# One move for both first units' x, tables and weight splits at other places, three runs of unread matmuls, and the last output groups two and two

## The chip, the cores and the metric

The kernel runs on one core of a Trainium2 chip. The metric is the device time of one execution in microseconds (us); less is better. Engines are TensorE (PE in the profile; PEld is its weight load), VectorE (DVE), ScalarE (ACT), GpSimd (POOL) and SyncE (SP), which only issues DMAs here.

## The reference

A gated linear attention over 4 batches, 8 heads, 768 tokens and head size 48; then a mixture of 4 experts over its 3072 x 384 output; then a gated feed-forward layer.

```python
for t in range(S):
    state = alpha[:, :, t, :, None] * state + np.einsum('bhd,bhe->bhde', k[:, :, t], v[:, :, t])
    y[:, :, t] = np.einsum('bhd,bhde->bhe', q[:, :, t], state)
...
p = domain_probs / (domain_probs.sum(-1, keepdims=True) + 1e-09)
for e in range(E):                       # E = 4, w1[e] 384 x 1024, w2[e] 1024 x 384
    h = np.maximum(x @ w1[e], 0.0)
    out += p[:, e:e + 1] * (h @ w2[e])
...
h = x @ w_in                             # 384 x 2048
g = h - np.tanh(h)
return (g @ w_out).astype(np.float32)    # 2048 x 384
```

## The kernel before

**Attention.** Tokens are cut into 12 units u of 256 tokens; each is worked through in 17 steps (`attention(u, step)`). Products of decays at three levels (`tabulate`, nine tables on the way) scale queries (`spread_queries`, `spread_distant`, `rotate`) and keys (`raise_keys`), so that TensorE can form the scores of a chunk (`diagonal`, `scores(u, level, half)`). DVE picks the valid ones with copy_predicated (`pick`). `turn` transposes keys, `deltas` forms each chunk's part of the state, `states` on DVE adds them up in time, `carry_own` copies the states beside the values, and `attend` gives the outputs, which are x for the next stage. Scores and tables lie in two sets of buffers: set 1 (names ending in b) is for unit 1 alone, set 0 for all others. Units 0 and 1 (`AHEAD = 2`) run ahead of everything; the rest are interleaved with the feed-forward part, unit 2m+2 from slot 0 of block m and unit 2m+3 from slot 16. Steps are one to a slot.

**x.** An fp32 product is made from three fp32r products of high and low parts, so each operand is split: the high part is a copy (ScalarE: `high_x`, `split_high`, `hidden_high`), the low one a subtraction (DVE: `low_x`, `split_low`, `hidden_low`; GpSimd makes some of the weights'). `attend` leaves 128 of 384 features of x in 16-row pieces at the wrong place; they go through the buffer XS and are moved by DMAs (`move`, `move_half`), three pieces kt with two halves of the rows each.

**Feed-forward.** Tokens go in 6 blocks m of 512; each has 32 slots s of the experts and 16 slots f of the last layer. A slot is `first` (x times a 384 x 128 weight block, nine products of 512 columns) and, four slots later, `second` (the hidden block times the next weights). DVE scales the hidden block (`scale`). In the last layer `cube` and ScalarE's `functions` form g, and `second2` adds into four output tiles t. Weights come from DRAM by SP (`stage(g)`, four staging buffers WS), are split into the ring RG, and saved for the later blocks (`save`).

**Order.** Each engine's program is written out by hand; engines meet by semaphores. `w_low` counts the weight splits' low parts in order, whoever makes them: splits 0 and 1 are GpSimd's, 2 to 5 DVE's, then 6 and on GpSimd's. GpSimd waits with split 6 until `w_low` is 6:

```python
def split_low(g):                         # on GpSimd
    if g == LEAD + 2:                     # LEAD = 4
        pool.wait_ge(w_low, g)
    pool.wait_ge(w_high, g + 1)
...
def attention(u, step):                   # on GpSimd
    if step in (3, 6, 9):
        raise_keys(u, step // 3 - 1)
```

TensorE's `scores(u, level, half)` with level 1 wait for `keys_up`, which `raise_keys` counts; `first(m, s)` waits for `scaled` of slot s - 2; `scores(2, 0, 1)` waits for the picks of `scores(2, 0, 0)`.

Of the kernel before, what the change touches and what calls it, by code (L numbers as in the profile page):

```python
# [7 lines left out]
fp32 = mybir.dt.float32  # L8
f32r = mybir.dt.float32r
# [8 lines left out]
P = 128  # L18
CH = 64
# [66 lines left out]
def own(u):  # L86

    return int(u == 1)
# [6 lines left out]
def turn_of(u):  # L95

    return len(same_set(u))
# [21 lines left out]


def carried_at(u):
    return 4 * (turn_of(u) + 1)
# [18 lines left out]
def program(nc, qka_d, v_d, dp_d, w1_d, w2_d, win_d, wout_d, mask_d, ones_d, ident_d, out_d):  # L141
    ctx = ExitStack()
    with ctx:
# [45 lines left out]
        T64 = [place(f"T64_{n}", CHUNKS) for n in range(2)]  # L189
        XS = [place("XS", 2 * UT, f32r), place("XSb", 2 * UT, f32r)]  # L190

# [13 lines left out]
        def sems(name):  # L205
            return sem(name), sem(name + "_b")
# [17 lines left out]
        x_low = sems("x_low")  # L224
        moved = [sems(f"moved{j}") for j in range(KT)]

# [82 lines left out]
        def to_move(u, j, hh):  # L309

            src = XS[own(u)][CH * hh + SPARE * j:CH * hh + SPARE * (j + 1), :].rearrange("p (h t) -> p h t", h=2)
            dst = x_tile(u)[CH * hh + D:CH * hh + CH, :, j, x_tokens(u)]
            return dst.bitcast(fp32), src.bitcast(fp32)

        def state_slot(u, c):
# [26 lines left out]
        def _(sp):  # L342
# [12 lines left out]
            def move(u):  # L355
                for j in (2, 0, 1):
                    sp.wait_ge(x_low[own(u)], 3 * turn_of(u) + (2 if j == 2 else 3))
                    for hh in range(1 if u == 1 else 2):
                        dst, src = to_move(u, j, hh)
                        sp.dma_start(dst, src).then_inc(moved[j][own(u)], 16)  # L360

# [90 lines left out]
            for g in range(2):  # L452
                stage(g + STAGES)
            move(0)
            move(1)
            for g in range(2, LEAD):
# [24 lines left out]
        def _(pe):  # L481
# [89 lines left out]
            def attend(u, n):  # L571
# [10 lines left out]
                last.then_inc(filled[own(u)], 1)  # L582

            def attention(u, step):
                if step == 0:
                    diagonal(u)
                if step in (1, 2):
                    scores(u, 0, step - 1)
                if step in (4, 5):
                    scores(u, 1, step - 4)  # L590
                if step in (7, 8):
                    scores(u, 2, step - 7)
                if step == 10:
# [25 lines left out]
            def first_product(m, g, out, x_moved=False, x_mixed=False):  # L619
                order = (2, 0, 1) if x_moved else (0, 1, 2)  # L620
                for kt in order:
                    if x_moved:
                        for u in (2 * m, 2 * m + 1):
                            pe.wait_ge(moved[kt][own(u)], 32 * turn_of(u) + 32)
                    if x_mixed:
                        pe.wait_ge(x2_low, KT * m + kt + 1)
                    nc.tensor.matmul(out, w1(g, 0, kt), x_part(m, 0, kt), start=(kt == order[0]), stop=False)  # L627
                    nc.tensor.matmul(out, w1(g, 0, kt), x_part(m, 1, kt), start=False, stop=False)  # L628
                    last = nc.tensor.matmul(out, w1(g, 1, kt), x_part(m, 0, kt), start=False, stop=(kt == order[-1]))  # L629
                last.then_inc(hid, 1)  # L630
# [73 lines left out]
            pe.wait_ge(prob_step, E + 2)  # L704
            nc.tensor.transpose(bank[3][0:E * NTB * TT, 0:P], prob[:, :], ident[:, :]).then_inc(prob_turned, 1)
            deltas(1, 0)
            deltas(1, 1)
            attend(0, 0)
            pe.wait_ge(prob_laid, 1)
            attend(0, 1)  # L710
            attend(1, 0)
            attend(1, 1)
            diagonal(AHEAD)
            for m in range(NTB):
                for s in range(SLOTS1):
# [15 lines left out]
                for f in range(SLOTS2):  # L731
                    first2(m, f)
                    if f >= LEAD:
                        second2(m, f - LEAD)
            for t in range(TT):
                for f in range(SLOTS2 - LEAD, SLOTS2):
                    second2(NTB - 1, f, [t])
# [3 lines left out]
        def _(act):  # L741
# [52 lines left out]
            def high_x(u):  # L794
                x, t = x_tile(u), x_tokens(u)
                if u // 2 >= 2:
                    act.wait_ge(hid, SLOTS * (u // 2 - 1))
                act.wait_ge(filled[own(u)], filled_at(u, 18))
                if turn_of(u):
                    for j in range(KT):  # L800
                        act.wait_ge(moved[j][own(u)], 32 * turn_of(u))
                nc.scalar.activation(XS[own(u)][:, 0:UT], fill_bank(u, 18)[:, UT:2 * UT], ACT.Copy).then_inc(x_high[own(u)], 1)
                nc.scalar.activation(x[:, 0, 2, t], fill_bank(u, 18)[:, 0:UT], ACT.Copy).then_inc(x_high[own(u)], 1)
                act.wait_ge(filled[own(u)], filled_at(u, 19))
                nc.scalar.activation(x[:, 0, 0:2, t], fill_bank(u, 19)[:, :].rearrange("p (a t) -> p a t", a=2),
                                     ACT.Copy).then_inc(x_high[own(u)], 1)

            def move_half(u):
                for j in (2, 0, 1):
                    act.wait_ge(x_low[own(u)], 3 * turn_of(u) + (2 if j == 2 else 3))  # L810
                    dst, src = to_move(u, j, 1)
                    act.dma_start(dst, src).then_inc(moved[j][own(u)], 16)

# [75 lines left out]
            high_x(1)  # L889
            move_half(1)  # L890
            split_high(LEAD)
# [24 lines left out]
        def _(dve):  # L916
# [95 lines left out]
            def low_x(u):  # L1012
                x, t = x_tile(u), x_tokens(u)
                dve.wait_ge(x_high[own(u)], 3 * turn_of(u) + 2)
                nc.vector.tensor_tensor(XS[own(u)][:, UT:2 * UT], fill_bank(u, 18)[:, UT:2 * UT], XS[own(u)][:, 0:UT].bitcast(fp32),
                                        ALU.subtract).then_inc(x_low[own(u)], 1)
# [180 lines left out]
            rotate(AHEAD, 0)  # L1197
            split_low(LEAD)
            split_low(LEAD + 1)
            for m in range(NTB):  # L1200
                for s in range(SLOTS1):
# [5 lines left out]
                    for u, step in units_at(m, s):  # L1207
                        attention(u, step)
                low_x2(m)
                for f in range(SLOTS2):  # L1210
# [9 lines left out]
        def _(pool):  # L1220
# [24 lines left out]

            def prepare(u):
                n = turn_of(u)
# [4 lines left out]
                tabulate(u, 0, 1)  # L1252
                spread_queries(u)
                spread_distant(u)
                tabulate(u, 1, 9)
# [34 lines left out]
            split_low(1)  # L1290
            pool.wait_ge(carried[1], carried_at(1))
            prepare(2)
            split_low(LEAD + 2)
# [45 lines left out]
```

## Time and profile before

| | us |
|---|---|
| median of 3 runs | 1391.01 |
| lowest and highest | 1390.82, 1391.07 |
| the profiled execution | 1391.59 |
| its span in the trace | 1389.8 |
| PE busy | 1346.7 (97%) |
| DVE busy | 873.0 (63%) |
| ACT busy | 559.8 (40%) |
| POOL busy | 274.0 (20%) |

All times of the trace count from the start of the span. A row of a timeline has the start, the time from the first start to the last end of the instructions merged in it, engine, line, operation and tile, their number, and in brackets how long the engine was idle before it and what released it. Records of fp32 products come in pairs, so x64 are 32 products.

### The profile page before, as it was taken

What the parts mean: (1) busy time and instruction counts of PE and PEld (TensorE: products, weight loads), DVE (VectorE), ACT (ScalarE), POOL (GpSimd) and SP (SyncE); (2) the same over time, 40 slices, a digit from 0 to 9 for tenths busy, and PEclk for the clock granted to TensorE, in tenths of its full rate; (3) what the DMA queues carried; (4) which work ended last, traced back from release to release, by engine and by line L of the source; (5) the groups of instructions that cost most, each with busy time, mean ns of one, the idle gap of its engine ahead of it and who ended that gap; (6) DMA issues with size and microseconds to landing.
All of it is one profiled execution on the core that took longest, in us unless ns stands there. A gap on an engine that the chain in (4) does not pass through costs nothing.

```text
span 1389.8 us, 25813 instructions
## 1 busy us (share of the span) xinstructions
PE 1346.7 (97%) x10177; PEld 1130.4 (81%) x10177; DVE 873.0 (63%) x1763; ACT 559.8 (40%) x1002; POOL 274.0 (20%) x272
## 2 busy tenths in 40 slices
PE   3599999999999999999999999999999999999998
PEld 3578788988878888878898887898887889888887
DVE  8884855994654875465687565497556378333385
ACT  1525346843213751313662323374231376111185
POOL 4566655004022001313001403000221000000000
PEclk8799999999999999999999999999999999999999
DMA  7389696966655656565755655665664465655552
GB/s 214 90 307 319 235 327 232 325 211 220 205 197 190 233 181 219 177 211 193 241 183 180 219 195 194 206 229 169 221 204 166 159 221 189 217 191 195 193 192 70
DMA packets 104968, 289.08 MB, mean 208 GB/s; under 512 B 10032, under 2 KB 64912, under 8 KB 104848
## 3 DMA queue, kind: packets, MB, share of 16 engines
q1 hardware_dynamic: 104704, 287.33, 61.6%
q8 instruction: 81, 1.33, 0.4%
q14 instruction: 39, 0.32, 0.1%
q10 hardware_dynamic: 144, 0.10, 0.0%
HBM read 242.52 MB, written 42.52 MB: 205 GB/s over the span
## 4 chain that ended last, share of the span: by engine, by line
PE 88%; DVE 6%; issue 3%; POOL 2%; ACT 1%; DMA 0%; DVEq 0%; POOLq 0%; ACTq 0%
PE bank L627 14%; PE bank L628 13%; PE bank L629 13%; PE bank L652 9%; PE bank L653 9%; PE bank L654 9%; PE bank L676 4%; PE bank L678 4%; PE bank L677 4%; PE bank L542 3%; PE bank L579 1%; PE bank L566 1%; DVE RG L1110 1%; DVE GG L1080 1%; PE bank L520 1%
## 5 line engine op out<-in xcount | busy, mean ns | idle before, releaser
L839 ACT ACTIVATE HH<-GG 128x512 fp32r<-128x512 f32 x192 | 121.2, 631 | 654.5 <-PE bank L654 529.1
L627 PE MATMUL bank<-XB,RG 128*128 128x512 f32 x864 | 349.8, 405 | 3.8 <-DMA XB<-XSb 3.5
L628 PE MATMUL bank<-XB,RG 128*128 128x512 f32 x864 | 340.7, 394 | 0.0
L629 PE MATMUL bank<-XB,RG 128*128 128x512 f32 x864 | 339.7, 393 | 0.0
L1053 DVE SCALAR_TENSOR_TENSOR GG<-bank,PB 128x512 f32<-128x512 f32 x192 | 133.3, 695 | 318.1 <-PE bank L629 317.9
L652 PE MATMUL bank<-HH,RG 128*128 128x512 f32 x576 | 224.6, 390 | 0.0
L653 PE MATMUL bank<-HH,RG 128*128 128x512 f32 x576 | 224.5, 390 | 0.0
L654 PE MATMUL bank<-HL,RG 128*128 128x512 f32 x576 | 224.3, 389 | 0.0
L1264 POOL TENSOR_TENSOR KU<-KU,TOT 128x256 f32<-128x256 f32 x88 | 68.5, 805 | 704.2 <-PE bank L542 704.2
L627 PEld LDWEIGHTS bank<-XB,RG 128*128 128x128 f32 x864 | 162.9, 189 | 44.6 <-issue 3.6
L629 PEld LDWEIGHTS bank<-XB,RG 128*128 128x128 f32 x864 | 162.9, 189 | 35.4
L628 PEld LDWEIGHTS bank<-XB,RG 128*128 128x128 f32 x864 | 163.1, 189 | 28.7
L1059 DVE TENSOR_TENSOR HL<-GG,HH 128x512 fp32r<-128x512 f32 x192 | 159.1, 828 | 8.9 <-ACT HH L839 8.8
L949 DVE COPY_PREDICATED SC<-masks,bank 128x192 f32<-128x192 int32 (+2 forms) x396 | 98.8, 357 | 67.5 <-PE bank L542 67.2
L676 PE MATMUL bank<-RG,HH 128*128 128x384 f32 x384 | 129.7, 338 | 1.5 <-DVE HL L1089 1.4
L678 PE MATMUL bank<-RG,HL 128*128 128x384 f32 x384 | 129.7, 338 | 0.0
L677 PE MATMUL bank<-RG,HH 128*128 128x384 f32 x384 | 129.1, 336 | 0.0
L652 PEld LDWEIGHTS bank<-HH,RG 128*128 128x128 f32 x576 | 108.2, 188 | 23.0
L654 PEld LDWEIGHTS bank<-HL,RG 128*128 128x128 f32 x576 | 108.2, 188 | 22.5
L653 PEld LDWEIGHTS bank<-HH,RG 128*128 128x128 f32 x576 | 108.2, 188 | 22.5
L1076 DVE TENSOR_TENSOR GG<-SQ,bank 128x512 f32<-128x512 f32 x96 | 65.7, 684 | 39.7 <-ACT TH L849 39.7
L848 ACT ACTIVATE SQ<-bank 128x512 f32<-128x512 f32 x96 | 57.1, 595 | 67.4 <-PE bank L629 66.3
(129 smaller groups left out, 1654.4 us busy)
## 6 DMA issues: line engine op xcount, KB each, us to landing
RG<-scratch SPq DMA_DIRECT2D x240, 768.0 KB, 4.3
scratch<-RG SPq DMA_DIRECT2D x48, 768.0 KB, 5.2
VS<-vp SPq DMA_DIRECT2D x11, 768.0 KB, 6.0
WS<-w SPq DMA_DIRECT2D x32, 192.0 KB, 3.1
PB<-probs SPq DMA_DIRECT2D x6, 1024.0 KB, 6.8
AU<-qka SPq DMA_DIRECT2D x11, 512.0 KB, 5.4
R<-qka SPq DMA_DIRECT2D x11, 512.0 KB, 5.2
KU<-qka SPq DMA_DIRECT2D x11, 512.0 KB, 6.2
```

Of the source, the lines that this page charges most:

```text
L627: nc.tensor.matmul(out, w1(g, 0, kt), x_part(m, 0, kt), start=(kt == order[0]), stop=False)
L628: nc.tensor.matmul(out, w1(g, 0, kt), x_part(m, 1, kt), start=False, stop=False)
L629: last = nc.tensor.matmul(out, w1(g, 1, kt), x_part(m, 0, kt), start=False, stop=(kt == order[-1]))
L652: nc.tensor.matmul(out, w2(g, 0)[:, c], HH[:, h_slot(g)], start=(s == 0), stop=False)
L653: nc.tensor.matmul(out, w2(g, 1)[:, c], HH[:, h_slot(g)], start=False, stop=False)
L654: return nc.tensor.matmul(out, w2(g, 0)[:, c], HL[:, h_slot(g)], start=False, stop=(s == SLOTS1 - 1))
L676: nc.tensor.matmul(out, HH[:, h], w2(g, 0), start=(f == 0), stop=False)
L677: nc.tensor.matmul(out, HH[:, h], w2(g, 1), start=False, stop=False)
L678: last = nc.tensor.matmul(out, HL[:, h], w2(g, 0), start=False, stop=(f == SLOTS2 - 1))
L839: nc.scalar.activation(HH[:, h_slot(g)], GG[:, h_slot(g)], ACT.Copy).then_inc(high, 1)
L1053: nc.vector.scalar_tensor_tensor(GG[:, h_slot(g)], h_bank[s % 2][:, :], 0.0, PB[:, e * TB:e * TB + TB], op0=ALU.max, op1=ALU.mult).then_in ...
L1059: nc.vector.tensor_tensor(HL[:, h_slot(g)], GG[:, h_slot(g)], HH[:, h_slot(g)].bitcast(fp32), ALU.subtract).then_inc(low, 1)
```

## The change

Seven edits. (1) XS becomes one buffer that holds both first units' parts side by side, and one set of three moves for each half of the rows (`move_first`, on SP and on ScalarE's queue) takes both units' x at once, where SP issued nine and ScalarE three. A move now waits for both units. (2) The counter of moves is one for each kt. (3) TensorE gets 12, 8 and 8 fp32 products of 128 columns that nothing reads (`keep_clock`), after the transpose of the probabilities, after attend(0, 1) and after the diagonal of unit 2. (4) GpSimd begins unit 2's tables when DVE has made rotate(1, 2), and waits for the carry copies of unit 1 between the spreading of queries and the distant queries. (5) DVE makes splits 4 and 5 behind the steps of slots 1 and 2 of block 0. (6) In the last block's last four slots f, the first two are added into all four output tiles, then the last two tile by tile. (7) Later units use the first quarter and the third of XS.

```diff
-        XS = [place("XS", 2 * UT, f32r), place("XSb", 2 * UT, f32r)]
+        XS = place("XS", 2 * AHEAD * UT, f32r)
...
+        def to_move_first(j, hh):
+
+            src = XS[CH * hh + SPARE * j:CH * hh + SPARE * (j + 1), :].rearrange("p (h w) -> p h w", h=2)
+            dst = x_tile(0)[CH * hh + D:CH * hh + CH, :, j, :]
+            return dst.bitcast(fp32), src.bitcast(fp32)
...
+            def move_first():
+                for j in (2, 0, 1):
+                    for u in range(AHEAD):
+                        sp.wait_ge(x_low[u], 2 if j == 2 else 3)
+                    dst, src = to_move_first(j, 0)
+                    sp.dma_start(dst, src).then_inc(moved[j], 16)
...
-            move(0)
-            move(1)
+            move_first()
...
+            def keep_clock(out, n):
+
+                for i in range(n):
+                    nc.tensor.matmul(out[:, 0:P], ident[:, :], ident[:, :], start=True, stop=True)
...
+            keep_clock(bank[2], 12)
             deltas(1, 0)
...
             attend(0, 1)
+            keep_clock(bank[7], 8)
             attend(1, 0)
             attend(1, 1)
             diagonal(AHEAD)
+            keep_clock(bank[4], 8)
...
+            for f in range(SLOTS2 - LEAD, SLOTS2 - 2):
+                second2(NTB - 1, f)
             for t in range(TT):
-                for f in range(SLOTS2 - LEAD, SLOTS2):
+                for f in range(SLOTS2 - 2, SLOTS2):
                     second2(NTB - 1, f, [t])
...
-            move_half(1)
+            move_first()
...
             rotate(AHEAD, 0)
-            split_low(LEAD)
-            split_low(LEAD + 1)
             for m in range(NTB):
                 for s in range(SLOTS1):
                     scale(m, s)
...
+                    if m == 0 and s in (1, 2):
+                        split_low(s + LEAD - 1)
...
                 tabulate(u, 0, 1)
                 spread_queries(u)
+                if pause:
+                    pool.wait_ge(carried[own(u - 1)], pause)
                 spread_distant(u)
...
-            pool.wait_ge(carried[1], carried_at(1))
-            prepare(2)
+            pool.wait_ge(rotated[1], 3)
+            prepare(2, carried_at(1))
             split_low(LEAD + 2)
```

DVE before, from the last products of rotate(2, 0) on: RG4 and RG5 are the low parts of weights 4 and 5, GG the scaled hidden block, HL its low part, SC the picked scores.

```order
L295 TENSOR_TENSOR R1_83<-R1_83,TOT_96 128x64x4
L1110 TENSOR_TENSOR RG4_61<-WS0_65,RG4_61 128x2x384
L1110 TENSOR_TENSOR RG5_62<-WS1_66,RG5_62 128x2x384
L1053 SCALAR_TENSOR_TENSOR GG_71<-bank0,PB_54 128x512
L1053 SCALAR_TENSOR_TENSOR GG_71<-bank1,PB_54 128x512
L1059 TENSOR_TENSOR HL_70<-GG_71,HH_69 128x512
L949 COPY_PREDICATED SC_87<-masks_50,bank5 128x64x3
```

DVE at the same place now, to the second split:

```order
L299 TENSOR_TENSOR R1_83<-R1_83,TOT_96 128x64x4
L1084 SCALAR_TENSOR_TENSOR GG_71<-bank0,PB_54 128x512
L1084 SCALAR_TENSOR_TENSOR GG_71<-bank1,PB_54 128x512
L1090 TENSOR_TENSOR HL_70<-GG_71,HH_69 128x512
...
L980 COPY_PREDICATED SC_87<-masks_50,bank6 128x64
L1141 TENSOR_TENSOR RG4_61<-WS0_65,RG4_61 128x2x384
L1084 SCALAR_TENSOR_TENSOR GG_71<-bank0,PB_54 128x512
L1090 TENSOR_TENSOR HL_70<-GG_71,HH_69 128x512
...
L980 COPY_PREDICATED SC_87<-masks_50,bank6 128x64
L1141 TENSOR_TENSOR RG5_62<-WS1_66,RG5_62 128x2x384
```

Both splits moved behind the first scalings: the first behind two scalings, a low part and six picks, the second behind a scaling, a low part and six picks more.

GpSimd now, from the last table of unit 2 on, with what each waits for; the order of these is as before. RG_63 and RG_64 are splits 6 and 7, the three KU are raise_keys(2, 0).

```order
L1264 TENSOR_TENSOR TOT<-TOT 128x32 [waits tabled]
L1264 TENSOR_TENSOR T_0_98<-TOT 128x16 [waits tabled]
L1310 TENSOR_TENSOR RG_63<-WS_67,RG_63 128x2x384 [waits w_high,w_low]
L1310 TENSOR_TENSOR RG_64<-WS_68,RG_64 128x2x384 [waits w_high]
L1297 TENSOR_TENSOR KU<-KU,TOT 128x256 [waits tabled,filled]
L1297 TENSOR_TENSOR KU<-KU,TOT 128x256
L1297 TENSOR_TENSOR KU<-KU,AU 128x256
```

What moved here is not a row but what it waits for: w_low reaches 6 with DVE's split of RG5, above.

## Rows read from the trace of the kernel before

**Rows 1.** The page's 40 slices of the span, TensorE, busy share in tenths

```profile
PE   3599999999999999999999999999999999999998
```

**Rows 2.** Windows: stretch, length, busy by engine, granted clock, DMA share, GB/s

```profile
53.00:54.00 1.00, 0.34 (x5) 0.31 (x7) 1.00 (x6) 0.95 (x3) 0.54 (x1) 0.62 0.00 0
...
66.00:67.00 1.00, 0.00 (x0) 0.00 (x0) 1.00 (x1) 0.10 (x1) 1.00 (x2) 0.95 0.23 49
73.00:74.00 1.00, 1.00 (x4) 0.76 (x4) 1.00 (x3) 0.00 (x0) 0.92 (x2) 0.64 0.35 102
```

**Rows 3.** Timeline of TensorE, 53 to 87 us

```profile
53.66 2.98 PE L566 MATMUL bank<-VSb,KJb 64*48 64x48 f32 x64 [3.41 <-DVE SCb L949]
...
64.59 0.27 PE L520 MATMUL bank<-R,KU 64*64 64x64 f32 x1 [1.85 <-issue]
68.33 0.76 PE L627 MATMUL bank<-XB,RG 128*128 128x512 f32 x1 [3.48 <-DMA XB<-XSb]
...
75.14 0.89 PE L542 MATMUL bank<-R,KU 64*64 64x96 f32 x32
...
78.92 0.89 PE L542 MATMUL bank<-R,KU 64*64 64x96 f32 x32 [0.61 <-DVE SC L949]
...
86.09 0.89 PE L542 MATMUL bank<-R,KU 64*64 64x96 f32 x32
```

**Rows 4.** Timeline of DVE, 53 to 90 us

```profile
53.56 1.09 DVE L976 TENSOR_TENSOR R2b<-R2b,TOTb 128x256 f32<-128x256 f32 x3
55.49 2.89 DVE L1000 SCALAR_TENSOR_TENSOR ST<-ST,T,bank 112x48 f32<-112x48 f32 x16 [0.84 <-PE bank L566]
58.41 0.94 DVE L1010 COPY VSb<-ST 48x576 f32<-48x576 f32 x2
...
68.61 0.40 DVE L968 COPY R<-R 128x256 f32<-128x256 f32 x1 [1.28 <-POOL TOT L1233]
...
73.03 1.93 DVE L1110 TENSOR_TENSOR RG<-WS,RG 128x768 fp32r<-128x768 f32 x2
...
76.86 1.92 DVE L949 COPY_PREDICATED SC<-masks,bank 128x192 f32<-128x192 int32 x6
...
88.28 1.28 DVE L949 COPY_PREDICATED SC<-masks,bank 128x192 f32<-128x192 int32 x6
```

**Rows 5.** GpSimd: timeline, and two lines' instructions (ns min/median/max)

```profile
59.43 2.12 POOL L1233 TENSOR_TENSOR TOT<-AU 128x768 f32<-128x768 f32 x1 [5.89 <-DVE VSb L1010]
...
77.10 3.65 POOL L1277 TENSOR_TENSOR RG<-WS,RG 128x768 fp32r<-128x768 f32 x2 [2.95 <-ACT RG L831]
...
83.17 1.18 POOL L1264 TENSOR_TENSOR KU<-KU,AU 128x256 f32<-128x256 f32 x1
...
L1233 POOL TENSOR_TENSOR TOT<-AU x10: 1467/1468/2117, 59.4 to 1005.1; 128x768 f32<-128x768 f32 x10
...
L1264 POOL TENSOR_TENSOR KU<-KU,TOT x88: 625/700/1550, 16.2 to 1079.5; 128x256 f32<-128x256 f32 x88
```

**Rows 6.** Timeline of DVE and GpSimd, 11 to 15 us

```profile
11.59 2.38 POOL L1238 TENSOR_TENSOR R0b<-R1b,AUb 128x1024 f32<-128x1024 f32 x1 [11.14 <-DMA R1b<-qka]
12.59 1.63 DVE L968 COPY R<-R 128x256 f32<-128x256 f32 x1
```

**Rows 7.** Timeline of the queues of SP and ScalarE, the moves

```profile
61.47 4.74 SPq L360 DMA_DIRECT2D XB<-XS  x6
62.27 2.21 ACTq L812 DMA_DIRECT2D XB<-XSb  x3
66.25 1.86 SPq L360 DMA_DIRECT2D XB<-XSb  x3
```

**Rows 8.** Timeline of TensorE, the last block's last groups

```profile
1379.12 0.44 PE L676 MATMUL bank<-RG,HH 128*128 128x384 f32 x1 [1.44 <-DVE HL L1089]
...
1380.57 0.34 PE L676 MATMUL bank<-RG,HH 128*128 128x384 f32 x1
...
1381.09 0.33 PE L676 MATMUL bank<-RG,HH 128*128 128x384 f32 x1
```

More of the change, by code:

```diff
@@ L118, in stated_at, with moved_at @@
     return PG * (sum(states_in(v) for v in same_set(u)) + c)
+def moved_at(u):
+    return 32 * max(1, u)
 def carried_at(u):
@@ L224, in program @@
         x_low = sems("x_low")
-        moved = [sems(f"moved{j}") for j in range(KT)]
+        moved = [sem(f"moved{j}") for j in range(KT)]
         prob_step = sem("prob_step")
@@ L309, in to_move, with x_aside @@
         def to_move(u, j, hh):
-            src = XS[own(u)][CH * hh + SPARE * j:CH * hh + SPARE * (j + 1), :].rearrange("p (h t) -> p h t", h=2)
+            src = XS[CH * hh + SPARE * j:CH * hh + SPARE * (j + 1), :].rearrange("p (h w) -> p h w", h=2)[:, :, 0:UT]
             dst = x_tile(u)[CH * hh + D:CH * hh + CH, :, j, x_tokens(u)]
             return dst.bitcast(fp32), src.bitcast(fp32)
+        def to_move_first(j, hh):
+            src = XS[CH * hh + SPARE * j:CH * hh + SPARE * (j + 1), :].rearrange("p (h w) -> p h w", h=2)
+            dst = x_tile(0)[CH * hh + D:CH * hh + CH, :, j, :]
+            return dst.bitcast(fp32), src.bitcast(fp32)
+        def x_aside(u, part):
+            at = part * AHEAD * UT + own(u) * UT
+            return XS[:, at:at + UT]
         def state_slot(u, c):
@@ L357, in move @@
                     sp.wait_ge(x_low[own(u)], 3 * turn_of(u) + (2 if j == 2 else 3))
-                    for hh in range(1 if u == 1 else 2):
+                    for hh in range(2):
                         dst, src = to_move(u, j, hh)
-                        sp.dma_start(dst, src).then_inc(moved[j][own(u)], 16)
+                        sp.dma_start(dst, src).then_inc(moved[j], 16)
[4 more added lines that the diff above has]
+                    dst, src = to_move_first(j, 0)
+                    sp.dma_start(dst, src).then_inc(moved[j], 16)
             def attention(u, step):
@@ L622, in first_product @@
                     if x_moved:
-                        for u in (2 * m, 2 * m + 1):
-                            pe.wait_ge(moved[kt][own(u)], 32 * turn_of(u) + 32)
+                        pe.wait_ge(moved[kt], moved_at(2 * m + 1))
                     if x_mixed:
@@ L798, in high_x @@
                 act.wait_ge(filled[own(u)], filled_at(u, 18))
-                if turn_of(u):
+                if u >= AHEAD:
                     for j in range(KT):
-                        act.wait_ge(moved[j][own(u)], 32 * turn_of(u))
-                nc.scalar.activation(XS[own(u)][:, 0:UT], fill_bank(u, 18)[:, UT:2 * UT], ACT.Copy).then_inc(x_high[own(u)], 1)
+                        act.wait_ge(moved[j], moved_at(u - 1))
+                nc.scalar.activation(x_aside(u, 0), fill_bank(u, 18)[:, UT:2 * UT], ACT.Copy).then_inc(x_high[own(u)], 1)
                 nc.scalar.activation(x[:, 0, 2, t], fill_bank(u, 18)[:, 0:UT], ACT.Copy).then_inc(x_high[own(u)], 1)
@@ L806, in high_x, with move_first @@
                                      ACT.Copy).then_inc(x_high[own(u)], 1)
-            def move_half(u):
+            def move_first():
                 for j in (2, 0, 1):
-                    act.wait_ge(x_low[own(u)], 3 * turn_of(u) + (2 if j == 2 else 3))
-                    dst, src = to_move(u, j, 1)
-                    act.dma_start(dst, src).then_inc(moved[j][own(u)], 16)
+                    for u in range(AHEAD):
+                        act.wait_ge(x_low[u], 2 if j == 2 else 3)
+                    dst, src = to_move_first(j, 1)
+                    act.dma_start(dst, src).then_inc(moved[j], 16)
             def attention(u, step):
@@ L1014, in low_x @@
                 dve.wait_ge(x_high[own(u)], 3 * turn_of(u) + 2)
-                nc.vector.tensor_tensor(XS[own(u)][:, UT:2 * UT], fill_bank(u, 18)[:, UT:2 * UT], XS[own(u)][:, 0:UT].bitcast(fp32),
+                nc.vector.tensor_tensor(x_aside(u, 1), fill_bank(u, 18)[:, UT:2 * UT], x_aside(u, 0).bitcast(fp32),
                                         ALU.subtract).then_inc(x_low[own(u)], 1)
@@ L1244, in spread_distant, with prepare @@
                 distant(nc.gpsimd, u, 0).then_inc(spread[own(u)], 1)
-            def prepare(u):
+            def prepare(u, pause=0):
                 n = turn_of(u)
```

## Prediction

> **What bounds the kernel now.** I read the page's slices first: TensorE stands at 9 tenths in every slice but the first and the last [rows 1], so a microsecond counts only if TensorE would have waited, or run at its lower clock, in it. Both happen at the front (before about 80 us) and at the end. Everything between is TensorE's own work, with DVE, ScalarE and the queues beside it, and just shifts.
>
> Front, in TensorE's timeline [rows 3]. The transpose of the probabilities is over at 50.25; the deltas of unit 1 come at 53.66 after 3.41 idle, when DVE has picked the last score of SCb. The diagonal of unit 2 has 63 of its 64 records by about 62.7 and the last at 64.59, after 1.85 with no releaser. The first product of the feed-forward part starts at 68.33, 3.48 after that, when a move of XSb has landed. Then come scores(2,0,0) at 75.14, scores(2,0,1) at 78.92 (0.61 idle, for DVE) and scores(2,1,0) at 86.09, from where TensorE no longer waits.
>
> The clock [rows 2]: it falls from 1.00 (2.4 GHz) to 0.50 (1.2 GHz) once the 3.4 us gap has nearly passed (mean of 53 to 54: 0.62, so at about 53.4), and again at 66.95 in the gap before the first product (mean of 66 to 67: 0.95); it is back at 1.00 in 73 to 74 (0.64, so at 73.7 at the latest, by the pace of the products 73.6). Of the first two products, 5.3 us (68.33 to 73.6) ran at half speed, 2.6 us more than at full.
>
> DVE [rows 4] is as busy as TensorE there: rotate(1,2) until 54.65, states of unit 1 until 58.38, its two carry copies until 59.35, a weight split, then x; then the diagonal's picks, a split, the rotation of unit 2 from 68.61, two more splits until 74.96, and only then the scaling of the first hidden block, without which the third product cannot start. GpSimd [rows 5] starts unit 2's tables at 59.43, after 5.89 idle for the carry copies; DVE's rotation waits 1.28 for them [rows 4]. It ends raise_keys(2,0) at 84.35 (83.17 + 1.18), and scores(2,1,0) needs that: 1.7 us of slack to 86.09.
>
> **The tail.** The last group has two waits for DVE: 1.44 before 1379.12, and between 1379.12 and 1380.57 two groups of three products took 1.45 where one group back to back takes 0.52 (1380.57 to 1381.09) [rows 8]. The new order puts products of f = 12 and 13 for all four tiles first: eight groups of three, of which two ran before the first wait. The other six are 6 x 0.52 = 3.1 us of work with nothing to wait for, and what it waits for (f = 14 by 1379.1, f = 15 by 1379.9) is then long there. Lost before: 1.44 + (1.45 - 1.04) = 1.85; I take **1.9** (bounds 1.6, if the new group starts have a cost of their own, and 2.0). The last tile's drain and store stay last and are not changed; the other tiles' stores now come 1.0 us apart instead of 2.1, still more than a drain takes.
>
> **The clock fillers.** Each is a 128x128 fp32 product. No row has one. The nearest are the deltas of unit 1 at half clock: 64 records of 48 columns, two side by side, in 2.98, so 0.093 for 48 columns; 128 columns in two records are 2 x 2.67 x 0.093 = 0.50 at half clock and 0.25 at full [rows 3]. Twelve after the transpose: 50.25 + 3.0 = 53.25, inside the 3.41 us stand, so they cost nothing (at half clock, 6.0 us, they would end at 56.2 and delay). The clock is at 1.00 when they start and they fill the stand that lost it, so the deltas should run at full clock: 2.98 us becomes about 1.5. That gives DVE's states only what it waited for, 0.84 less ScalarE's carry: they would start with the end of rotate(1,2), at 54.9, and end at 54.9 + 2.89 = 57.8, some 0.6 us earlier. The eight after attend(0,1) take 2.0 us and are paid from the 1.5 us by which TensorE is ahead there and the wait for DVE's carry that it has anyway; the last eight fill the stand before the first product. The odd 1.85 us at 64.59 need not stay; if it does it hides behind the move.
>
> **Tables earlier.** GpSimd now starts when rotate(1,2) is done (54.65) instead of at 59.43: 1.47 for the first table (the undisturbed value; 2.12 was beside a DVE split) to 56.2, then the spreading of queries, 2.4 us for the same instruction of unit 1 [rows 6], to 58.6 [rows 5]. DVE's carry copies would start at 57.8. A DVE copy beside that instruction of unit 1 took 1.63 us, though another of its line took 0.40 [rows 4], and ended just after it (14.22 and 13.97) [rows 6], so the first copy ends near 59.0, the second at 59.5: x comes 0.1 to 0.2 us **later** than before, and the 0.6 is gone. GpSimd's distant queries and second table follow. Before, they ended when the rotation began, 68.6 - 59.4 = 9.2 after the start of the first table, 4.7 of it without that table and the spreading; so now they end at 59.5 + 4.7 = 64.2, and DVE's rotation no longer waits for them.
>
> The Trainium skill, page "SBUF — State Buffer", section "SBUF: two separate sides", has a rule for this that speaks against the change: the port pair that the two engines share is locked by whichever comes first, for its whole instruction. By it the copies wait for all of the spreading; with ports shared freely x would come 0.6 us earlier instead.
>
> **One move for both units.** Before, SP issued six moves of unit 0 (61.47 to 66.21) and then unit 1's; the one that released the product was issued at 66.25 and it started 2.1 later [rows 7]. Now SP and ScalarE's queue issue three each, the first when DVE has both units' third part, which is where ScalarE's queue began with unit 1's before, 62.27. 62.3 + 2.1 to 2.6 = 64.4 to 64.9, and the fillers end by 65.0. The first product starts near **65.0**, 3.3 us earlier, at full clock; the first two took 75.14 - 68.33 = 6.8, less 2.6 is 4.2, so they are over at 69.2, and scores(2,0,0) (0.89 [rows 3]) at 70.1.
>
> **Splits moved: who is next.** DVE now: pick of the diagonal to 64.3, split_low(3) to 65.3, rotation. It took 73.03 - 68.61 = 4.4 us beside the tables, and does again, with GpSimd's third and later tables beside it: 65.3 + 4.4 = **R = 69.7**. There the scaling starts, instead of at 74.96: 5.2 us earlier. TensorE, ready at 70.1, waits till 70.4 for it.
>
> Now the moved splits. GpSimd's split_low(6) stands ahead of raise_keys(2,0) in its program and waits for w_low = 6, that is for split_low(5), which DVE now does at the end of s = 2. From R: two scalings and the low part of block 0 take 2.0, as before (76.86 less 74.9), six picks 1.2 (the undisturbed six at 88.28), split_low(4) 0.9: 4.1. Then a scaling and a low part 1.2, six picks 1.2, split_low(5) 0.9: **7.4** [rows 4]. GpSimd: two splits of 1.82 (3.65 for both) to 11.1, raise_keys(2,0) 84.35 - 80.75 = 3.6 [rows 5] to 14.7; its three pieces undisturbed are 2 x 0.63 + 1.18 = 2.4, so 13.5 at the least. I take 14.2, beside DVE's rotation of level 1: keys at 83.9, scores(2,1,0) at **84.0**. TensorE issues scores(2,0,1) when the first picks are done, at R + 3.1 = 72.8, and from there it has the 86.09 - 78.92 = 7.2 us of work that it had before [rows 3]: ready at 80.0, it stands for 4.0 us. Against 86.09 the front is worth **2.0** us there (bounds 0.6, with R = 70.3 and 15.1, and 3.5, with 69.2 and 13.3). Behind it TensorE keeps its order; DVE is two splits later than before against it but had TensorE's stand of 4 us to make up for that. SP's stage(9) waits for w_low = 6 too, queued behind stage(8), five issues and a save later, so 77.1 should cost it nothing.
>
> A stand of 4.0 us is longer than the 3.41 that lost the clock [rows 2, 3]. If it does so here, about 3.2 us behind 84 run at half speed, a loss of 1.6. Nothing between 0 and 1.6 is shown; I take the middle, **0.8**.
>
> **Sum.** 1.9 + 2.0 - 0.8 = 3.1 us from the profiled 1391.59, which lies 0.6 above the median of the runs (1391.01): forecast 1391.0 - 3.1 = **1387.9**.
>
> **Rivals.**
> *Keys do not hold TensorE back.* If GpSimd's splits and keys are done by R + 10, the front is worth 86.09 - 80.0 = 6.1, with the tail 8.0: 1383.0; half of the wait left gives 1385.0. For it: DVE may reach split_low(5) sooner where GpSimd stands idle. Against: 3.65 + 2.4 behind 7.4 is already 13.5. Chance 0.17.
> *The clock is lost in full, or the tables cost more.* Front 2.0 - 1.6 or less, down to nothing when keys come at 86.1: 1388.3 to 1389.2. For it: the stand is longer than the one before the deltas. Chance 0.30. That the front gives nothing at all, because the product is held by something else until 86.1, is the end of this: 1389.1 by the tail alone.
> *Slower: fillers at half clock.* Should the granted clock be low when the twelve start, they end at 56.2, the deltas at 59.2 instead of 56.6, and eight more of 4.0 us, at half clock too, stand ahead of attend(1,0): unit 1's x some 6.6 us later or more. scores(2,1,0) at 84.0 + 6.6 = 90.6 instead of 86.1, 4.5, less the tail: 2.6 us slower, 1393.6, and 1395 with attend at half clock. It decides once x is later by more than the 2.1 us that the front has in hand and the 1.9 of the tail, so from 4 us. Against it: the mean of 0.62 in 53 to 54 has the fall inside it [rows 2], so the clock was full while the twelve would run, with less work than now. Chance 0.04.
>
> **How the numbers follow.** Forecast case (1.9 to 2.0 off at the end, keys the limit, clock in part): 0.49, own range 1386.2 to 1388.9. With the rivals at 0.17, 0.30 and 0.04, the range that leaves out no more than 2 in 10 is 1384.5 to 1390.3. 0.2% is 2.8 us, about what a measurement of this kernel tells from no change: below 1388.2 lie rival one and some 0.41 of the forecast case: faster 0.58; same 0.37; slower 0.05.
>
> **What would show it.** In the changed trace: deltas of unit 1 in about 1.6 us; no granted clock of 0.50 from 47 to 80; first product at 65; POOL's split of RG started only after DVE's second moved split, at about 77; TensorE idle about 4 us before scores(2,1,0), released by POOL's KU, and perhaps 0.50 behind it; no wait in the last group. The prediction is wrong if TensorE is not idle at that place, if the carry copies are not held by POOL, or if the first product starts later than 67.

## Result and profile after

Over 20 runs each the changed kernel took 1393.28 us (median, 1392.03 to 1398.03) against 1390.93 (1390.47 to 1391.76) before: ratio 1.0020, interval [1.0014, 1.0027]. It is **slower by 0.2%**, where 1387.9 was forecast, and lies outside the forecast range (1384.5 to 1390.3). The profiled execution took 1392.1 with a span of 1390.3, against 1391.59 and 1389.8.

Of the 2.35 us between the medians, 0.5 is in the two profiles. The rest comes from where each profiled execution lies among its runs: 0.7 above the median before, 1.2 below it now. The runs are 6 us wide now, 1.3 before. A second profile, further down, shows part of what moves.

TensorE's busy tenths in the 40 slices of the page, the row that answers to [rows 1]:

```profile
PE   3789999999999999999999999999999999999999
```

The front is fuller, but a busy TensorE is not one that gets on: 6.9 us of the new filling are the unread products, three rows of which follow below. The waits of TensorE (tile, line, releaser: us in total, times, longest):

```profile
PE bank L563 <- POOL KU L1297: 4.8, 1, 4.8
...
PE bank L652 <- DMA XB<-XS: 1.2, 1, 1.2
PE bank L600 <- issue: 0.9, 1, 0.9
...
PE bank L652 <- DMA RG<-scratch: 0.3, 1, 0.3
```

The wait of 3.5 for XSb and that of 1.4 in the last group are gone, that of 3.4 for SCb is 0.7; one of 4.8 us for GpSimd's raised keys is new. Where they stand, in TensorE's timeline (start, length, engine, line, operation, count, idle before), to be laid beside [rows 3]:

```profile
49.97 2.84 PE L608 MATMUL bank<-ident 128*128 128x128 f32 x24
...
57.40 0.26 PE L600 MATMUL bank<-R,VS 128*48 128x64 f32 x1 [0.93 <-issue]
...
58.21 2.05 PE L608 MATMUL bank<-ident 128*128 128x128 f32 x16
...
63.26 0.85 PE L541 MATMUL bank<-R,KU 64*64 64x64 f32 x41 [0.58 <-issue]
64.04 2.05 PE L608 MATMUL bank<-ident 128*128 128x128 f32 x16
67.31 0.47 PE L652 MATMUL bank<-XB,RG 128*128 128x512 f32 x1 [1.22 <-DMA XB<-XS]
...
74.95 0.89 PE L563 MATMUL bank<-R,KU 64*64 64x96 f32 x32 [0.20 <-DVE SC L980]
...
87.02 1.35 PE L563 MATMUL bank<-R,KU 64*64 64x96 f32 x32 [4.83 <-POOL KU L1297]
...
93.74 0.89 PE L563 MATMUL bank<-R,KU 64*64 64x96 f32 x32
```

scores(2,0,1) is 4.0 us earlier than before (74.95 for 78.92), scores(2,1,0) is 0.9 later (87.02 for 86.09), and scores(2,1,1) is 2.5 later (93.74 for 91.26). Before, it stood 5.2 behind scores(2,1,0):

```profile
91.26 0.89 PE L542 MATMUL bank<-R,KU 64*64 64x96 f32 x32
```

What lies between the last two now is the clock (window, length, TensorE busy, granted clock, DMA share, GB/s):

```profile
86.00:87.00 1.00, 0.00 (x0) 1.00 1.01 338
87.00:88.00 1.00, 0.98 (x31) 0.65 1.11 402
88.00:89.00 1.00, 1.00 (x14) 0.50 1.06 438
89.00:90.00 1.00, 1.00 (x4) 0.50 0.95 287
90.00:91.00 1.00, 1.00 (x4) 0.65 1.02 332
91.00:92.00 1.00, 1.00 (x6) 1.00 1.07 444
```

The stand ends, the clock falls from 2.4 to 1.2 GHz just as the work comes back (a mean of 0.65 in 87 to 88 puts the fall at 87.3), and 3.4 us run at half rate. The chain that leads to the stand, first on DVE, then on GpSimd:

```profile
70.02 0.69 DVE L1084 SCALAR_TENSOR_TENSOR GG<-bank,PB 128x512 f32<-128x512 f32 x1
71.70 0.69 DVE L1084 SCALAR_TENSOR_TENSOR GG<-bank,PB 128x512 f32<-128x512 f32 x1 [0.99 <-PE bank L654]
...
72.91 1.89 DVE L980 COPY_PREDICATED SC<-masks,bank 128x192 f32<-128x192 int32 x6
74.42 1.16 DVE L1141 TENSOR_TENSOR RG<-WS,RG 128x768 fp32r<-128x768 f32 x1
...
76.69 1.88 DVE L980 COPY_PREDICATED SC<-masks,bank 128x192 f32<-128x192 int32 x6
78.20 1.16 DVE L1141 TENSOR_TENSOR RG<-WS,RG 128x768 fp32r<-128x768 f32 x1
...
83.57 3.67 DVE L1004 TENSOR_TENSOR R<-R,TOT 128x256 f32<-128x256 f32 x3
```

```profile
79.44 4.06 POOL L1310 TENSOR_TENSOR RG<-WS,RG 128x768 fp32r<-128x768 f32 x2 [10.36 <-DVE RG L1141]
83.46 2.22 POOL L1297 TENSOR_TENSOR KU<-KU,TOT 128x256 f32<-128x256 f32 x2
85.63 1.33 POOL L1297 TENSOR_TENSOR KU<-KU,AU 128x256 f32<-128x256 f32 x1
```

GpSimd stands 10.36 us until DVE's split 5 is done at 79.36, then makes its two splits, and the keys are out at 86.96. Before, those two splits ran from 77.10 [rows 5].

The joint moves, in the queues of SP and ScalarE (compare [rows 7]), and the last group's drains on ScalarE:

```profile
62.86 3.41 SPq L382 DMA_DIRECT2D XB<-XS  x3
...
62.87 3.40 ACTq L843 DMA_DIRECT2D XB<-XS  x3
```

```profile
1384.47 0.49 ACT L903 ACTIVATE OUT<-bank 128x384 f32<-128x384 f32 x1 [2.74 <-PE bank L703]
...
1387.54 0.49 ACT L903 ACTIVATE OUT<-bank 128x384 f32<-128x384 f32 x1 [0.55 <-PE bank L703]
```

The last drain begins 2.8 us before the span's end, as its order demands, and is 0.5 later than before; the front is 2.5 later. The difference, 2.0, is what the tail gives.

### The profile page after: what moved, and what is told of

Read it like the earlier page. It is cut to its first block, busy times and chain, and to the rows that moved or that the text cites. A ratio compares the mean times of both kernels' runs of the same rounds, so it can differ in the third digit from the quotient of the medians.

```text
span 1390.3 us, 25908 instructions
## 1 busy us (share of the span) xinstructions
PE 1351.0 (97%) x10233; PEld 1134.6 (82%) x10233; DVE 873.9 (63%) x1763; ACT 560.0 (40%) x1002; POOL 273.1 (20%) x272
## 4 chain that ended last, share of the span: by engine, by line
PE 89%; DVE 7%; issue 2%; DMA 1%; POOL 1%; ACT 0%; DVEq 0%; SPq 0%; POOLq 0%
PE bank L652 14%; PE bank L653 13%; PE bank L654 13%; PE bank L677 9%; PE bank L678 9%; PE bank L679 9%; PE bank L703 4%; PE bank L701 4%; PE bank L702 4%; PE bank L563 4%; PE bank L600 2%; PE bank L587 1%; PE bank L541 1%; PE bank L576 1%; DVE RG L1141 1%
```

## Experiments

**Theories.** (A) The splits: split 5, done later by DVE, lets GpSimd's splits 6 and 7 start late, the raised keys behind them late, and TensorE stands and loses its clock. (B) The unread products: their 6.9 us of TensorE and the stall on issue push unit 1's attention and x back. (C) The early tables or the joint move lose more beside other work than they give. The runs of before beside the groups had medians of 1391.18, 1391.06 and 1391.06.

### Does the tail give 1.9, and do the splits alone cost?

tail_only is the kernel before with this edit:

```
+            for f in range(SLOTS2 - LEAD, SLOTS2 - 2):
+                second2(NTB - 1, f)
             for t in range(TT):
-                for f in range(SLOTS2 - LEAD, SLOTS2):
+                for f in range(SLOTS2 - 2, SLOTS2):
```

> The kernel before with the last output groups two and two, and nothing else. Theory (the tail gives its 1.9 us back and the loss is at the front): both waits for DVE in the last group are gone, 1389.0 to 1389.3 against 1391.0. Rival (the stores, now 1 us apart, hold each other up): the waits are gone but the time stays within 0.5 of before.

Measured: 1389.30 (1388.71 to 1389.84 in ten runs; an eleventh took 1911.87, and without it the median is 1389.19), ratio 0.9985 [0.9976, 0.9994]; span 1387.5 for 1389.8, and no wait in the last group. The term holds: 1.9 to 2.0 by the medians.

splits_only is the kernel before with this one:

```
-            split_low(LEAD)
-            split_low(LEAD + 1)
...
+                    if m == 0 and s in (1, 2):
+                        split_low(s + LEAD - 1)
```

> The kernel before with DVE's splits 4 and 5 behind slots 1 and 2, and nothing else. Theory (GpSimd's split 6 waits for split 5, and the raised keys stand behind it): split 5 ends near 83, keys near 90.5, so scores(2,1,0) starts 4 to 5 us later than 86.1, with the granted clock at 0.50 behind it for a few us: 1395 to 1397. Rival (the move only takes DVE work out of the way): within 0.5 of before or a little faster.

Measured: 1397.39 (1397.04 to 1397.61), ratio 1.0044 [1.0031, 1.0057]. TensorE's timeline, with the products at half rate behind the stand (granted clock 0.50 from 89 to 95):

```profile
88.64 1.56 PE L542 MATMUL bank<-R,KU 64*64 64x96 f32 x32 [4.83 <-POOL KU L1264]
...
96.72 0.89 PE L542 MATMUL bank<-R,KU 64*64 64x96 f32 x32
```

Nothing but the place of two DVE instructions is changed. scores(2,1,1) comes 5.5 us late (96.72 for 91.26), and the span is 5.4 longer. Of the 5.5, 2.6 are the late keys and 2.9 the half rate behind them. The expectation had more for the keys (at 90.5; they were out at 88.6), less for the clock, and the time lies just above its range. By (B) or (C) the two splits should have cost nothing.

### Taking the splits back

splits_back is the changed kernel with splits 4 and 5 ahead of slot 0 again (the last diff, reversed).

> The changed kernel with splits 4 and 5 back ahead of slot 0. Theory: no stand before scores(2,1,0), which starts near 82.4 instead of 87.0, and no 0.50 clock behind it: 1385.4 to 1386.5, and the spread of the changed kernel's runs shrinks. Rival (the fillers or the joint move are the loss): the stand only moves to another wait, 1390 or more.

Measured: 1387.11 (1385.65 to 1391.54), ratio 0.9979 [0.9970, 0.9988], 6 us under the changed kernel; span 1384.4. GpSimd's and TensorE's rows:

```profile
73.58 3.63 POOL L1310 TENSOR_TENSOR RG<-WS,RG 128x768 fp32r<-128x768 f32 x2 [3.83 <-ACT RG L862]
77.17 2.51 POOL L1297 TENSOR_TENSOR KU<-KU,TOT 128x256 f32<-128x256 f32 x2
79.65 1.17 POOL L1297 TENSOR_TENSOR KU<-KU,AU 128x256 f32<-128x256 f32 x1
```

```profile
82.56 0.89 PE L563 MATMUL bank<-R,KU 64*64 64x96 f32 x32
87.73 0.89 PE L563 MATMUL bank<-R,KU 64*64 64x96 f32 x32
```

The keys are out at 80.8, TensorE comes for them at 82.56 without a wait, at full clock. Against before, scores(2,1,1) is 3.5 early, and with the tail 5.4 are gained in the span. So the rest of the change gains, and the splits turned it round. The spread did not shrink as expected: 5.9 us over nine runs.

keys_first keeps the splits moved but breaks the chain at its other end, in GpSimd's program:

```
-            split_low(LEAD + 2)
-            split_low(LEAD + 3)
...
+                    if m == 0 and s == 3:
+                        split_low(LEAD + 2)
+                        split_low(LEAD + 3)
```

> The changed kernel with the splits still moved, but GpSimd makes raise_keys(2,0) before splits 6 and 7. Theory: keys are ready near 79.5 and scores(2,1,0) starts near 82.2: 1385 to 1386, like the kernel with the splits back, which shows that the order on GpSimd and not DVE's time is what costs. Rival (DVE itself is too late for TensorE with the splits moved): a stand of several us remains and the time is 1389 or more.

Measured: 1389.99 (1386.93 to 1394.62), ratio 0.9994 [0.9982, 1.0007]; span 1385.5. The keys, made from 75.39 on, hold nobody, and the stand of 4.83 is gone; it leaves another, of 1.99 (TensorE, then DVE):

```profile
81.55 0.89 PE L563 MATMUL bank<-R,KU 64*64 64x96 f32 x32
88.77 0.89 PE L563 MATMUL bank<-R,KU 64*64 64x96 f32 x32 [1.99 <-DVE SC L980]
```

```profile
84.08 1.08 DVE L1004 TENSOR_TENSOR R<-R,TOT 128x256 f32<-128x256 f32 x3
```

DVE, two splits behind, picks scores(2,1,0) only by 88.6. The prediction's "TensorE's stand of 4 us to make up for that" was right only while the stand was there. In the profiles this leaves the kernel 1.0 us behind splits_back at scores(2,1,1) and 1.1 in the span. The expected 1385 to 1386 was missed: the runs reach from 1386.93 to 1394.62, and their median lies where the rival had it (1389 or more). So the order on GpSimd is the larger part of what the moved splits cost (0.9994 against 1.0020 of the changed kernel, intervals apart), but not all of it. The rest, from 0.9994 to 0.9979 with the splits back, is DVE's lateness by the profiles; its size is not shown, as the intervals overlap.

### The unread products, the move and the tables, each taken from splits_back

The groups of runs were taken apart, so these kernels are compared through their ratios to before as well as by medians. sb_nofill drops all three keep_clock lines, sb_nomid only `keep_clock(bank[7], 8)`, sb_first12 keeps only the first twelve. sb_moveold has the separate moves of before; sb_poollate has GpSimd's tables late again:

```
-            pool.wait_ge(rotated[1], 3)
-            prepare(2, carried_at(1))
+            pool.wait_ge(carried[1], carried_at(1))
+            prepare(2)
```

> Splits back, and none of the 28 unread products. What is asked: where the spread of the changed kernel's runs (1392.0 to 1398.0, and 1385.7 to 1391.5 with the splits back, against 1390.6 to 1391.8 before) comes from. Theory (the 28 products push the place where TensorE waits for its next block of instructions from the diagonal of unit 2, where nothing is late, into attend of unit 0, where x waits behind it): spread back to about 1 us, and the first two products at half clock again, 1386.5 to 1388. Rival (the spread is from the joint move or the earlier tables): the spread stays at several us.

Measured: 1386.16 (1385.75 to 1388.08), ratio 0.9966 [0.9954, 0.9978]; span 1384.2. The spread is 2.3 us over six runs, less than with the products but not the 1 us expected.

> Splits back, and of the unread products only the first 12 and the last 8, none between attend(0, 1) and attend(1, 0). Theory (a late instruction block delays attend(1, 0) by all of the eight products behind it, 2.0 us): lowest time as with them, 1385.5 to 1386.5, spread smaller by 1 to 2 us. Rival (the eight in the middle keep the clock at 1.00 for the first product): 0.50 comes back before 70 and the time rises by 1 to 2 us.

Measured: 1386.57 (1385.63 to 1388.98), ratio 0.9969 [0.9956, 0.9981]; span 1383.8.

> The changed kernel with splits 4 and 5 back ahead of slot 0 and only the first twelve unread products. The twelve stand in a wait for the tables' inputs and cost TensorE nothing; without the last eight, 65 to 71 us may be at half rate, as it was with none of them (0.66 and 0.77). 1385.5 to 1387 us, so between the kernel without any product (1386.2) and that without the middle ones (1386.6); a result over 1388 would say that the last eight products carry weight.

Measured: 1386.74 (1385.94 to 1391.24), ratio 0.9976 [0.9967, 0.9985]; span 1384.5.

The windows of sb_nofill show what the products had been there for:

```profile
53.00:59.00 6.00, 5.87 (x122) 0.50 0.60 160
59.00:65.00 6.00, 3.58 (x140) 0.99 0.90 209
65.00:71.00 6.00, 5.77 (x18) 0.72 0.50 124
```

Without them unit 1's deltas and unit 0's attend run at half rate and so do the first feed-forward products, and the time is the same. DVE stands behind that work (carries, x, picks) and is no later for it: its first scaling starts at 71.25 here and at 71.36 in splits_back. Between these four kernels (splits_back, sb_nofill, sb_nomid, sb_first12) no difference is sure.

> Splits back, and the moves as before the change (nine on SP, three on ScalarE's queue, unit by unit). Theory: SP's ninth issue comes near 67, the first product near 67 to 68 instead of 65 to 67: 1387 to 1388.5, spread as with the joint move. Rival (the joint move is the cause of the spread, its 64 KB pieces landing after 2.4 to 4.3 us): spread 1 us.

Measured: 1387.10 (1385.99 to 1389.67), ratio 0.9973 [0.9963, 0.9983]. The profiled run is its slowest (span 1387.9; a wait of 2.8 for XSb, the clock at 0.55 in 68 to 71). By the medians the joint move gives nothing once the tables are early (1387.10 and 1387.11): DVE's rotation ends at 69.7 with either. Nor is it the cause of the spread: with the old moves the runs are still 3.7 wide. It may guard against a late landing, which is not shown: in this slowest run the product came at 68.16 for 65.78, and DVE then waited 0.65 and 1.28 for TensorE.

> Splits back, and GpSimd's tables of unit 2 begun only behind the carry copies, as before the change. Theory: carry copies free of GpSimd 0.2 us earlier or not at all, but DVE's rotation waits for the tables until about 68.5, so the scaling starts near 74.9 as before: 1387.5 to 1389, spread unchanged. Rival (the earlier tables cost more by holding DVE's copies than they bring): 1385.5 or less.

Measured: 1389.79 (1388.86 to 1390.39), ratio 0.9988 [0.9979, 0.9997]. That is about the time of the tail alone (1389.30), so with the splits in place the early tables are the part of the front that pays: 2.7 us by the medians, 1.3 by the means (1389.62 and 1388.32, the spread of splits_back being so much wider; the two intervals overlap). This profile is of the kernel's slowest run. DVE and TensorE with the tables late:

```profile
68.20 0.41 DVE L999 COPY R<-R 128x256 f32<-128x256 f32 x1 [2.30 <-POOL TOT L1264]
```

```profile
75.25 0.69 PE L652 MATMUL bank<-XB,RG 128*128 128x512 f32 x1 [3.86 <-DVE GG L1084]
```

x is early, the rotation waits 2.30 for the tables, and TensorE stands 3.86 for the first scaled block: the gain of the move, turned into a wait one step further on.

### The changed kernel again, and the products with the splits moved

> The changed kernel once more, unaltered, for a second profile and for its spread. If the spread belongs to the program, the runs lie again between about 1392 and 1398 us with a median near 1393.3. The stand of TensorE for the raised keys (4.8 us in the first profile) is there in every execution by the theory on the moved splits; what moves from run to run is then the landing of the joint moves (2.4 to 4.3 us in the first profile) and the stall on issue in front of the eight middle products (0.93 us). If the second profile is slower than the first (1392.1) and these two are the same, the spread comes from another place, and the views by stage show which.

Measured: 1393.80 (1390.92 to 1398.26), ratio 1.0023 [1.0013, 1.0033]; span 1391.9, 1.6 over the first profile. Its timeline:

```profile
86.89 1.56 PE L563 MATMUL bank<-R,KU 64*64 64x96 f32 x32 [4.83 <-POOL KU L1297]
...
94.78 0.89 PE L563 MATMUL bank<-R,KU 64*64 64x96 f32 x32
...
290.69 0.50 PE L652 MATMUL bank<-XB,RG 128*128 128x512 f32 x1 [1.17 <-DMA RG<-scratch]
```

Its granted clock, in windows as above:

```profile
86.00:87.00 1.00, 0.11 (x4) 0.53 1.05 338
...
92.00:93.00 1.00, 1.00 (x4) 0.55 0.96 357
```

The stand is the same, but the granted clock is at 0.50 from 86.1 to 92.9, where the first profile had it there from 87.3 to 90.7: scores(2,1,1) is 1.0 later than in the first profile, from a start 0.1 earlier. At the first weight refill of the next block TensorE then waits 1.17 where it waited 0.29. The two differences, 1.0 and 0.9, less 0.2 that only the first profile waits for DVE a little later, make 1.7, near the 1.6 us between the spans: the diagonal of the next block stands at 295.07 for 293.43, and from there the two run alike. My expectation, the landing of the moves or the stall on issue, was wrong: the wait for the moves was 1.1 and 1.2, and though the stall in attend was 0.2 here and 0.9 there, scores(2,1,0) started within 0.1.

no_fillers is the changed kernel without its three keep_clock lines.

> The changed kernel without the 28 unread products; moves, tables, splits and tail stay. By the theory on the moved splits the stand for the raised keys stays (4 to 5 us) and so does the second half rate stretch behind it, and the median stays above that of before: 1392 to 1393.5 us. If the unread products are what costs (their 7.0 us of TensorE, or the stall on issue that they bring forward), the stand shrinks or goes and the median falls to 1390 or less. If the products are also what spreads the runs, their width falls from 6.0 us to about 2, as it did in the kernel with the splits back (5.9 to 2.3); if the early tables are, it stays near 6.

Measured: 1392.95 (1391.04 to 1393.91), ratio 1.0011 [1.0002, 1.0019]; span 1391.9.

```profile
65.91 0.76 PE L652 MATMUL bank<-XB,RG 128*128 128x512 f32 x1 [1.62 <-DVE RG L1138]
...
88.45 1.56 PE L563 MATMUL bank<-R,KU 64*64 64x96 f32 x32 [4.83 <-POOL KU L1294]
```

The first product starts 1.4 us earlier, but at half rate, and scores(2,0,0) then comes 1.4 later than in the changed kernel (73.00 for 71.59). The keys come 1.4 later with it, and the same stand of 4.83 is there. The median is 0.85 below that of the changed kernel beside it, with overlapping intervals, and still above before: (B) can hold for that much at most, not for the loss of 6 that the splits explain.

fill_tail is the kernel before with the products and the tail alone.

> The kernel before with the 28 unread products and the last groups two and two; moves, tables and splits as before. The tail gives 1.9 us, as alone (1389.3). If the unread products stand in idle time and only hold the clock, the sum is 1389.3 less at most 0.8 us of half rate time: 1388.5 to 1389.3. If they delay the first move's product (the second eight cost 2.0 us before attend(1, 0)), it is 1389.5 to 1391. Width: 1 to 2 us if the early tables or the joint moves spread the runs, 4 or more if the products do.

Measured: 1389.69 (1388.94 to 1393.64), ratio 0.9996 [0.9987, 1.0005]. The products bring nothing over the tail alone (1389.30), and three of eleven runs lie above 1392.5. In the profile the first product starts at 69.62, 1.3 later than in [rows 3], and the time at half rate does not end, it moves: 0.58 in 65 to 68, 0.50 in 71 to 74.

## Why the prediction was wrong

Its mechanism was right: DVE's late split 5 holds GpSimd's splits and keys, and TensorE stands for the keys. The chain that leads there was mis-sized by 3.0 us, more than the 2.1 us that the front had in hand. Its terms in order:

- **Tail, 1.9.** Right: 1.9 to 2.0 by the runs of tail_only, 2.0 by the two profiles here.
- **Twelve products cost nothing; deltas in 1.5.** Right: 2.84 us for the twelve, deltas in 1.64 at full clock. That DVE gains nothing by it was right too: its carries end at 59.2, 59.4 before, 59.5 forecast (the copies held beside GpSimd: 1.52 for the two, 0.94 before [rows 4]).
- **Tables earlier.** Right: the rotation no longer waits for them, and sb_poollate gives the gain back.
- **Eight middle products "paid from the 1.5 us by which TensorE is ahead".** Wrong. The stall on issue of 1.85, expected behind the diagonal or gone, came as 0.93 inside attend(0,1) and 0.58 in the diagonal. The eight started at 58.21, attend(1,0) at 60.19 (59.66 before), and x of unit 1 was held by TensorE: ScalarE's high parts waited 1.19 for it, and DVE 0.71 for them. Cost at the move: 62.3 became 62.9.
- **Move in 2.1 to 2.6, first product at 65.0.** Wrong: issued at 62.9, SP's half landed 2.4 to 3.6 later and ScalarE's 3.8 to 4.3, first product at 67.31. The text's own mark for a failure (later than 67) was met.
- **R = 69.7.** Nearly: 70.02, but by luck. The rotation began at 66.42, not 65.3, and took 3.6, not 4.4. DVE does not wait for the product before R, so a product 2.3 us late did not move it.
- **w_low = 6 at R + 7.4.** This is the step that failed: R + 9.3 (79.36). I counted the first two scalings as DVE's work alone, 2.0. They waited 0.99 for TensorE, whose second product ended at 71.7, because the first had come late. Six picks took 1.5 each time, not 1.2, and a split 1.1, not 0.9. The 1.2 was read from the picks of a later score (88.28 in [rows 4]), which take 1.28 from first start to last end; the picks of scores(2,0,0) stand in the same rows (76.86) with 1.92, and have 1.89 now. GpSimd stood idle through both sets and both splits, so it is not what stretched them; what does was not shown.
- **Keys at R + 14.2.** R + 16.9: two splits 4.06, not 3.65, and raised keys 3.5, not 3.1. Altogether 0.3 + 1.9 + 0.4 + 0.4 = 3.0 us: keys at 87.0 instead of 83.9, 0.9 past the 86.1 at which TensorE came to scores(2,1,0) before. The front, forecast to be worth 2.0 there, lost 0.9.
- **Stand of 4.0.** 4.83, as TensorE came at 82.2, not 80.0. Here lies the trap of the sum: "worth 2.0 against 86.09" had a slack of 2.1 us to the point where the front turns to a loss, and the chain was 3.0 long in error. The bound of 15.1 for the keys was too tight.
- **Clock, 0.8 of 0 to 1.6.** All of it: 2.5 - 0.9 = 1.6 in the first profile, 3.5 - 0.8 = 2.7 in the second. The trace had shown the clock lost in a stand of 3.41, and a longer one was forecast; no row spoke for the middle. (The fall that the prediction puts at 53.4 lies at 53.2 by the mean of 0.62.)

Forecast to measured, at scores(2,1,1): 84.0 + 5.2 + 0.8 = 90.0 became 93.74, that is 3.0 for the chain and 0.7 for the clock. On the scale of the profiled executions the forecast was 1391.59 - 3.1 = 1388.5; with 3.7 it is 1392.2, and 1392.1 was measured. On the scale of the medians it is 1387.9 + 3.7 = 1391.6, and 1393.28 was measured: the 1.7 between them is the spread, of which the prediction had nothing.

**Rivals.** "Keys do not hold" came about in keys_first, where the keys were out at 79.0, and there DVE held TensorE in their place: median 1389.99, against its 1383.0 to 1385. With the splits put back it was 1386 to 1387. "Clock in full, or the tables cost more" had the clock right; its end, 1389.1, assumed that the front could not lose. "Fillers at half clock" was not what happened (1.00 while they ran). That the kernel came out slower, as this rival had it, is luck: it came about another way. What decided was the forecast's own chain, past its point of no gain; as a rival it would have been "keys past 86.1", and it had no chance of its own.

**Best kernel.** splits_back without the products has the lowest median, 1386.16, 0.34% under the kernel before, though no surely lower one than its three neighbours.

**Open.** The spread. Both causes seen in the two profiles lie behind the stand, yet splits_back and sb_first12 have no stand and still spread 5.9 and 5.3. The five kernels without unread products are 0.6 to 2.9 us wide, over 5 to 33 runs, and of the eight with them seven are 3.4 to 7.7 wide. So the products may well have a part in it, though the numbers of runs differ and a few runs show a narrower range; how was not shown. Of the seven wide kernels only sb_moveold has a profile of its slowest run, with the late move told above. Also open is why these six picks and the two moved splits take longer than those elsewhere in the kernel.

## What to carry to other kernels

A step moved out of one engine's way must be followed through the program order of the engine that waits for its count: here two 0.9 us splits, moved off DVE's path, held GpSimd's keys, which stood behind its own splits only by order. When a gain ends in a new stand, cost the chain to it with durations of the same instructions at the same step, not of like ones elsewhere, ask by how much it may be wrong before the sign turns, and take the lost clock as lost. Then follow the engine that got the moved work too: here it was the next to be late. Products that only hold the clock are worth trying only where TensorE's rate, and not another engine behind it, sets the next step.

## What the runs showed of the hardware

- Two engines side by side: DVE's three adds of the rotation took 3.67 us beside GpSimd's raised keys (83.57, above) and 1.08 in keys_first (84.08), where GpSimd stood idle from 84.0 on; just ahead of them GpSimd's two splits took 4.06, and 3.63 in splits_back. The Trainium skill, page "SBUF — State Buffer", section "SBUF: two separate sides", has an operation of DVE with two inputs in SBUF and one of GpSimd that reads there lock a shared port pair, each for its whole instruction; these rows agree: an add took 1.2, about as long as one of GpSimd's three (1.1 to 1.3).
- The idle time before the raised keys' product was 4.83 us in all four profiles that had it, though it began between 82.1 and 83.8; the work at half rate behind it was 3.4 us in one execution and 6.0 in another of the same program (4.0 in no_fillers, 6.4 in splits_only, by the granted clock). The fall itself came 5.1 and 4.0 us after TensorE's last product in the first two, 2.0 and 4.4 in the others.
- The stall on issue stands at other places when instructions are added ahead: 1.85 us in the diagonal before; 0.93 in attend and 0.58 in the diagonal with 28 products more; 0.56 and 1.89 in fill_tail; 1.60 in the diagonal in no_fillers. Its length also differs between executions of one program of TensorE: 0.2 and 0.49 in after_again, 0.9 and none in keys_first, 2.42 in splits_only for the 1.85 of before.
- Moves of 64 KB within SBUF, issued from 62.9 on, landed after 2.4 to 4.3 us; in splits_back the same moves took 2.3 to 3.5, and those of 32 KB before 2.0 to 3.3.
